# Up-projections by one level of Strassen's scheme over blocks of 384 tokens, with token-major down-projections weighted by a scalar

## The chip, the cores and the metric

The program runs on one core of a Trainium2 chip, as one launch from the inputs in the chip's memory (HBM) to the output there. A core has TensorE (PE; its weight loads are listed apart, PEld), VectorE (DVE), ScalarE (ACT), GpSimd (POOL) and SyncE (SP, which here only issues DMAs). Each engine works its own queue in order and waits for the others by semaphores. The metric is the device time in microseconds, the median of several runs.

## The reference

Three steps, all in float32; the output has 1536 tokens (2 x 768) by 512 features.

```python
# 1. attention: 2 batches, 8 heads, 768 tokens, head dimension 64; window of 128 and 4 sink tokens
scores = q @ k.T / sqrt(64)
keep = (pos_k < 4) | ((rel >= 0) & (rel < 128))        # rel = pos_q - pos_k
a = softmax(where(keep, scores, -1e9))
x = (a @ v), heads side by side: 1536 x 512
# 2. four experts, 512 -> 1024 -> 512, all of them for every token
p = domain_probs / (domain_probs.sum(-1) + 1e-9)
out = sum over e of p[:, e] * (relu(x @ w1[e]) @ w2[e])
# 3. second layer, 512 -> 2048 -> 512
h = out @ w_in
result = (h * cos(h)) @ w_out
```

## The kernel before

**Precision.** TensorE takes the reduced float32 form (fp32r) in one pass. Each operand of a projection is split into a high part, a cast (`x_hi`, `w1_hi`, `h_hi`, `w2_hi`), and a low part, the exact remainder (`x_lo` and so on), and each product is three matmuls: high x high, high x low, low x high.

**Attention.** 12 tiles of 128 tokens, 4 pairs of heads each, so `NP` = 48 steps j. Per step: scores on TensorE, masking and row maximum on VectorE (L624, L640), exponential on ScalarE (L491), normalising on VectorE (L679), a transpose of the weights, a split into two triangles on GpSimd (L386, L389), and the product with the values. The result of a tile is copied to `x_full` (L480) and split into `x_hi` (ScalarE) and `x_lo` (GpSimd L376). Between these steps the same queues load and split the first expert's weights: SP issues 256 KB of w1 and 256 KB of w2 for each of 8 chunks between the loads of keys, queries and values (`load_weights`, L276 and L279), VectorE casts w1 (L740), ScalarE casts w2, GpSimd takes both low parts.

**Projections.** A unit is one expert (1024 hidden features) or half of the second layer: `UNITS` = 6. Each unit has `STEPS` = 24 steps, 3 groups of 512 tokens by 8 chunks of 128 hidden features. In step s `up` computes one bank of 128 features x 512 tokens by 12 matmuls (4 parts of the contraction x 3, L962 to L964), two steps ahead (`LAG`), in three rotating banks. ScalarE writes `h_hi` with relu (L512), VectorE `h_lo` (L748), and `down_expert` adds 12 matmuls (L1013 to L1015: feature-major result, weights stationary) to four banks. After 8 chunks, VectorE multiplies each bank by the routing weight of each token, spread over all partitions in `probs_wide` (L775, into `routed`), and GpSimd adds it to `acc` (L433). `probs_wide` comes by a store of the routing to memory and a broadcast load of 3 MB.

**Second layer.** The same with `down` (L1032 to L1035, token-major: `h` is stationary) and a gate in place of relu: h/(2 pi) + 0.25 on ScalarE (L594, `turns`), rounding and its subtraction on VectorE (L804, L807, `frac`), sine on ScalarE (L602, `cosine`), product with h on VectorE (L819, `gated`), high part on ScalarE (L598), low part on VectorE (L812). `acc` of the experts is feature-major already and is only split into `x_hi` (L581) and `x_lo` (L440). The results are added to `acc` (L784) and stored, 12 x 256 KB (L331).

**Weights.** The next unit's chunks are loaded into four raw buffers each and split in the last third of a unit: high parts on ScalarE (L567, L571), w1's low parts on GpSimd (L424), w2's on VectorE (L761).

**Order.** Every queue is written out by hand. TensorE's is, per step, `up(u, s + LAG)` and then the down part of step s. Nothing is scheduled at run time.

## Time and profile before

| | us |
|---|---|
| runs | 917.54, 918.05, 912.59; median 917.54 |
| the profiled execution, first to last instruction | 918.1 |
| attention, until the matmuls of the projections run densely | 0 to 137 |
| expert projections | 137 to about 650 |
| second layer | about 650 to 915 |
| last accumulation and store | 915 to 918.1 |

All times are microseconds unless marked ns. Matmuls are pipelined and their records overlap, so what counts is the distance between their starts. The clock rows give the granted TensorE clock, full being 2.4 GHz and 0.5 being 1.2 GHz. Where two rows of the profile name an engine after "<-", that one ended the wait.

### The profile page before, as it was taken

To read this page: it belongs to the slowest core of one execution; us is meant where nothing else is said; L and a number is where in the kernel's file an instruction comes from. 1 tells how busy PE (TensorE), PEld (TensorE's weight loads), DVE (VectorE), ACT (ScalarE), POOL (GpSimd) and SP (SyncE) were. 2 spreads that over 40 slices of the span, in tenths; PEclk is the share of its full clock that TensorE was granted. 3 is DMA by queue.
4 is the path that set the end of the run, shared out by engine and by line. 5 is a ranking of instruction groups with operands and counts; after the bars stand their busy time and mean duration, and the time that the engine had idled before them with its cause. 6 is when DMAs were issued, how large, how long until landed. Compare 5 with 4: busy or idle time off the path is not lost.

```text
span 918.1 us, 12079 instructions
## 1 busy us (share of the span) xinstructions
PE 896.5 (98%) x4414; PEld 728.4 (79%) x4414; DVE 391.8 (43%) x892; ACT 277.0 (30%) x634; POOL 205.0 (22%) x226
## 2 busy tenths in 40 slices
PE   7889899999999999999999999999999999999998
PEld 5666578888888888888888888888788888888886
DVE  5887941312341213331214322133555456645454
ACT  5766641111221112311112211213343345333332
POOL 2564732103220204220204121235320012000000
PEclk9887989999999999999999999999999999999999
DMA  8355306000230000320001310002300002001011
GB/s 179 77 134 131 84 13 230 1 1 12 72 101 0 0 0 21 104 57 0 0 11 46 91 35 1 0 12 69 92 12 0 1 12 81 1 0 46 1 47 46
DMA packets 75020, 41.81 MB, mean 46 GB/s; under 512 B 42464, under 2 KB 67040, under 8 KB 74848
## 3 DMA queue, kind: packets, MB, share of 16 engines
q1 hardware_dynamic: 74976, 41.23, 16.4%
q8 instruction: 26, 0.43, 0.2%
q14 instruction: 18, 0.15, 0.1%
HBM read 37.79 MB, written 3.17 MB: 45 GB/s over the span
## 4 chain that ended last, share of the span: by engine, by line
PE 92%; DVE 5%; issue 1%; DMA 1%; ACT 0%; SPq 0%; ACTq 0%
PE scores L962 14%; PE scores L964 14%; PE scores L963 14%; PE bank L1015 9%; PE bank L1014 9%; PE bank L1013 9%; PE bank L1032 5%; PE bank L1035 5%; PE bank L1034 5%; DVE weights L679 2%; PE scores L899 2%; PE bank L933 2%; DVE scores L624 1%; PE bank L910 1%; DMA k_nat<-in_k_dram 1%
## 5 line engine op out<-in xcount | busy, mean ns | idle before, releaser
L962 PE MATMUL scores<-x_hi,w_hi 128*128 128x512 f32 x576 | 224.6, 390 | 0.0
L964 PE MATMUL scores<-x_hi,w_lo 128*128 128x512 f32 x576 | 224.1, 389 | 0.0
L963 PE MATMUL scores<-x_lo,w_hi 128*128 128x512 f32 x576 | 224.1, 389 | 0.0
L748 DVE SCALAR_TENSOR_TENSOR h_lo<-scores,h_hi 128x512 fp32r<-128x512 f32 x96 | 66.3, 691 | 361.4 <-ACT h_hi L512 361.4
L512 ACT ACTIVATE h_hi<-scores 128x512 fp32r<-128x512 f32 x96 | 57.4, 598 | 415.6 <-PE scores L964 415.6
L1013 PE MATMUL bank<-h_hi,w_hi 128*128 128x512 f32 x384 | 149.4, 389 | 0.0
L1014 PE MATMUL bank<-h_lo,w_hi 128*128 128x512 f32 x384 | 149.4, 389 | 0.0
L1015 PE MATMUL bank<-h_hi,w_lo 128*128 128x512 f32 x384 | 149.4, 389 | 0.0
L962 PEld LDWEIGHTS scores<-x_hi,w_hi 128*128 128x128 f32 x576 | 108.1, 188 | 22.7 <-issue 0.5
L964 PEld LDWEIGHTS scores<-x_hi,w_lo 128*128 128x128 f32 x576 | 108.2, 188 | 22.5
L963 PEld LDWEIGHTS scores<-x_lo,w_hi 128*128 128x128 f32 x576 | 108.1, 188 | 22.4
L424 POOL TENSOR_TENSOR w_lo<-w_raw,w_hi 128x512 fp32r<-128x512 f32 x40 | 51.5, 1289 | 276.9 <-ACT w_hi L567 276.9
L433 POOL TENSOR_TENSOR acc<-acc,routed 128x512 f32<-128x512 f32 x48 | 62.3, 1329 | 194.1 <-DVE routed L775 194.1
L1013 PEld LDWEIGHTS bank<-h_hi,w_hi 128*128 128x128 f32 x384 | 72.1, 188 | 15.0
L1014 PEld LDWEIGHTS bank<-h_lo,w_hi 128*128 128x128 f32 x384 | 72.1, 188 | 15.0
L1015 PEld LDWEIGHTS bank<-h_hi,w_lo 128*128 128x128 f32 x384 | 72.0, 188 | 14.9
L1032 PE MATMUL bank<-w_hi,h_hi 128*128 128x512 f32 x192 | 75.0, 391 | 0.0
L1035 PE MATMUL bank<-w_hi,h_lo 128*128 128x512 f32 x192 | 74.7, 389 | 0.0
L1034 PE MATMUL bank<-w_lo,h_hi 128*128 128x512 f32 x192 | 74.7, 389 | 0.0
L804 DVE TENSOR_SCALAR frac<-turns 128x512 f32<-128x512 f32 x48 | 21.3, 444 | 110.2 <-ACT turns L594 110.2
L594 ACT ACTIVATE turns<-scores 128x512 f32<-128x512 f32 x48 | 28.7, 598 | 129.5 <-PE scores L964 129.5
L491 ACT ACTIVATE weights<-masked,neg_max 128x132 f32<-128x132 f32 (+1 forms) x96 | 38.0, 397 | 38.7 <-DVE neg_max L640 37.5
(93 smaller groups left out, 931.5 us busy)
## 6 DMA issues: line engine op xcount, KB each, us to landing
w_raw<-in_moe_w_dram SPq DMA_DIRECT2D x64, 256.0 KB, 2.9
w_raw<-in_moe_w_in_dram SPq DMA_DIRECT2D x16, 256.0 KB, 3.1
w_raw<-in_moe_w_out_dram SPq DMA_DIRECT2D x16, 256.0 KB, 2.7
v_nat<-in_v_dram SPq DMA_DIRECT2D x12, 256.0 KB, 3.1
probs_wide<-routing_dram SPq DMA_DIRECT2D x1, 3072.0 KB, 11.3
out_dram<-acc SPq DMA_DIRECT2D x12, 256.0 KB, 2.1
k_nat<-in_k_dram SPq DMA_DIRECT2D x11, 256.0 KB, 5.0
q_nat<-in_q_dram SPq DMA_DIRECT2D x11, 256.0 KB, 5.4
```

The costliest lines, as they stand in the source:

```text
L433: nc.gpsimd.tensor_tensor(acc[:, g, c], acc[:, g, c], routed[:, c], ALU.add)\
L512: nc.scalar.activation(h_hi[:, s % U_BANKS, :], up_bank[s % U_BANKS][:], ACT.Relu)\
L748: nc.vector.scalar_tensor_tensor(h_lo[:, s % U_BANKS, :], up_bank[s % U_BANKS][:], 0.0, h_hi[:, s % U_BANKS, :].bitcast(F32), ALU.max, ALU ...
L962: nc.tensor.matmul(ub[:], w1_hi[:, f, c, :], x_hi[:, c, rows], start=(c == 0), stop=False)
L963: nc.tensor.matmul(ub[:], w1_hi[:, f, c, :], x_lo[:, c, rows], start=False, stop=False)
L964: last = nc.tensor.matmul(ub[:], w1_lo[:, f, c, :], x_hi[:, c, rows], start=False, stop=(c == KC - 1))
L1013: nc.tensor.matmul(down_bank[c][:], w2_hi[:, f, feats], h_hi[:, slot], start=(f == 0), stop=False)
L1014: nc.tensor.matmul(down_bank[c][:], w2_hi[:, f, feats], h_lo[:, slot], start=False, stop=False)
L1015: last = nc.tensor.matmul(down_bank[c][:], w2_lo[:, f, feats], h_hi[:, slot], start=False, stop=(f == FC - 1))
L1032: nc.tensor.matmul(down_bank[i][:], h_hi[:, slot, toks], w2_hi[:, f], start=(f == 0), stop=False)
L1034: nc.tensor.matmul(down_bank[i][:], h_hi[:, slot, toks], w2_lo[:, f], start=False, stop=False)
L1035: last = nc.tensor.matmul(down_bank[i][:], h_lo[:, slot, toks], w2_hi[:, f], start=False, stop=(f == FC - 1))
```

## The change

**Tiling.** The work is cut into `NS` = 24 stages of 768 tokens (one batch) and 512 hidden features: block 0 is the experts over batch 0 (stages 0 to 7), block 1 the experts over batch 1 (8 to 15), blocks 2 and 3 the second layer over batch 0 (16 to 19) and batch 1 (20 to 23), called gated stages.

**Up-projection.** In a stage, x (512 x 768) and w1 (512 x 512) are 2 x 2 matrices of blocks, 384 tokens being half the token side. Seven block products in Winograd's form of Strassen's scheme replace eight. A stage has two halves, a and b (h = 2s, 2s + 1), each of 128 of the 256 features of a block; `product(h, n)` is one of the seven for a half: 6 matmuls of 384 columns. The sums of weight blocks are made on GpSimd (`sum_weights`, 4 of 512 elements per partition and stage), those of token blocks too (`sum_tokens`, 4 of 768 per block of stages). The sums of products are made by letting products accumulate in a bank one after another (`chain_bank`: 1, 6, 5, 3; `side_bank`: 7, 4; `two_bank`: 2), and by copying the bank in between to SBUF on ScalarE (`keep_1`, `keep_2`, `keep_3` into `kept`) and adding the copy on VectorE to another bank or into `c22` (`add_11`, `add_22`, `add_21`). The next product into the chain bank waits for the copy. Each half yields four quarters, 11, 22, 12, 21, of 128 features x 384 tokens, which go through relu or the gate in pieces of 384 columns. `kept` and `c22` exist once: `keep_2(h)` waits until `add_21(h - 1)` is done.

**Down-projection.** Always token-major, as 6 tiles of 128 tokens x 512 features; `down(s, k, i)` is 6 matmuls for tile `DOWN_ORDER[k]` from half i, 72 matmuls per stage. It waits for the low parts of two quarters of its half. VectorE then adds each tile to `acc` (`keep_down`), for experts times the routing weight as a scalar per partition. The routing broadcast, its store and GpSimd's additions are gone.

**Between the layers.** `acc` is token-major now, so TensorE transposes it for the second layer (`turn_down`, 12 tiles x 4, at the ends of stages 8 to 10 and 16 to 18), VectorE copies the result to `x_t`. All seven token blocks of the next block of stages are split at the end of stages 7, 15 and 19 (`tokens_hi` on ScalarE and `tokens_lo` on VectorE, 7 x 768 columns each). The attention stage no longer splits x per tile; instead, the four token sums of batch 0 and their splits run one per step j from 30 to 42, and the weight sums and splits of stage 0 from 12 to 22 (splits of x and w1 on GpSimd and ScalarE).

**Weights.** Loads are 1 MB each, w1 and w2 once per stage, behind the stage before's last split. In an expert stage ScalarE splits the next stage's w1 after `relu_hi(b, 12)` and at the end, in a gated stage after the seventh cosine and at the end; w2 is split in the same stage (`second_hi`, `second_lo`, 2 x 1024 columns).

The diff cut to its core (helpers, names and the unchanged attention left out):

```diff
+        chain_bank = (bank[0], bank[3])
+        side_bank = (bank[1], bank[4])
+        two_bank = (bank[2], bank[5])
+        down_bank = (bank[6], bank[7], bank[2], bank[0], bank[1], bank[5])
+        x2_bank = (bank[6], bank[7])
...
-            def load_weights(first, second, u, f):
-                if not (isinstance(u, int) and RAW > u * FC + f):
-                    sp.wait_ge(w1_lo_ready, u * FC + (f - RAW + 1))
-                sp.dma_start(w1_raw[:, f % RAW], first).then_inc(w1_landed[f % RAW], 16)
-                if not (isinstance(u, int) and RAW > u * FC + f):
-                    sp.wait_ge(w2_lo_ready, u * FC + (f - RAW + 1))
-                sp.dma_start(w2_raw[:, f % RAW], second).then_inc(w2_landed[f % RAW], 16)
...
+            def load_first(s):
+                if s >= 1:
+                    sp.wait_ge(w1_lo_ready, 6 * s)
+                sp.dma_start(w1_raw[:], weights_of(s)[0].rearrange("(k p) f -> p k f", p=P)).then_inc(w1_landed, 16)
+            def load_second(s):
+                if s >= 1:
+                    sp.wait_ge(w2_lo_ready, 2 * s)
+                sp.dma_start(w2_raw[:], weights_of(s)[1].rearrange("(c p) d -> p c d", p=P)).then_inc(w2_landed, 16)
...
+            def sum_weights(s, n):
+                low, high = slice(0, FS // 2), slice(FS // 2, FS)
+                a11, a12 = w1_raw[:, 0:2, low], w1_raw[:, 2:4, low]
+                a21, a22 = w1_raw[:, 0:2, high], w1_raw[:, 2:4, high]
+                s2, s3, s4 = (w1_sum[:, i] for i in range(3))
+                if n == 0:
+                    pool.wait_ge(w1_landed, 16 * (s + 1))
+                    if s >= 1:
+                        pool.wait_ge(w1_lo_ready, 6 * s)
+                    nc.gpsimd.tensor_tensor(s3, a11, a21, ALU.subtract).then_inc(w1_summed, 1)
+                elif n == 1:
+                    pool.wait_ge(w1_summed, 4 * s + 1)
+                    nc.gpsimd.tensor_tensor(a21, a21, a22, ALU.add).then_inc(w1_summed, 1)
+                elif n == 2:
+                    pool.wait_ge(w1_summed, 4 * s + 2)
+                    nc.gpsimd.tensor_tensor(s2, a21, a11, ALU.subtract).then_inc(w1_summed, 1)
+                else:
+                    pool.wait_ge(w1_summed, 4 * s + 3)
+                    nc.gpsimd.tensor_tensor(s4, a12, s2, ALU.subtract).then_inc(w1_summed, 1)
...
+            for s in range(NS):
+                if s + 1 < NS:
+                    for n in range(4):
+                        sum_weights(s + 1, n)
+                if s + 2 in FIRST[1:3] or s + 1 == FIRST[3]:
+                    for n in range(4):
+                        sum_tokens(block_of(s) + 1, n)
+                if s + 1 < NS:
+                    for h in (2 * s + 2, 2 * s + 3):
+                        for part in range(3):
+                            first_lo(h, part)
...
+            def keep_2(h):
+                act.wait_ge(product_done[6], h + 1)
+                if h >= 1:
+                    act.wait_ge(c21_ready, h)
+                nc.scalar.activation(kept[:, 1], chain_bank[h % 2][:, 0:HALF], ACT.Copy).then_inc(kept2, 1)
...
+            def gated_hi(n):
+                h, c = 2 * FIRST[2] + n // 4, (11, 22, 12, 21)[n % 4]
+                act.wait_ge(gated_ready, n + 1)
+                act.wait_ge(down_done, TPB * (h // 2))
+                nc.scalar.activation(h_part(h_hi, h % 2, c), gated[:, n % 2], ACT.Copy).then_inc(hi_ready[c], 1)
...
+                a, b = 2 * s, 2 * s + 1
+                n = 8 * (s - FIRST[2])
+                if s >= 1:
+                    keep_1(a)
+                second_hi(s, 0)
+                if s >= 1:
+                    keep_2(a)
+                if is_gated(s):
+                    turn(n)
+                    keep_3(a)
+                    cosine(n)
+                    keep_1(b)
+                    turn(n + 1)
+                    gated_hi(n)
+                    cosine(n + 1)
+                    second_hi(s, 1)
+                    turn(n + 2)
+                    gated_hi(n + 1)
+                    cosine(n + 2)
+                    keep_2(b)
+                    turn(n + 3)
+                    gated_hi(n + 2)
+                    cosine(n + 3)
+                    turn(n + 4)
+                    keep_3(b)
+                    gated_hi(n + 3)
+                    cosine(n + 4)
+                    for m in range(n + 5, n + 8):
+                        turn(m)
+                        gated_hi(m - 1)
+                        cosine(m)
+                        if s + 1 < NS and m == n + 6:
+                            for part in range(3):
+                                first_hi(a + 2, part)
+                    gated_hi(n + 7)
+                else:
+                    relu_hi(a, 11)
+                    keep_3(a)
+                    keep_1(b)
+                    relu_hi(a, 22)
...
+                else:
+                    relu_hi(a, 11)
+                    keep_3(a)
+                    keep_1(b)
+                    relu_hi(a, 22)
+                    second_hi(s, 1)
+                    relu_hi(a, 12)
+                    keep_2(b)
+                    relu_hi(a, 21)
+                    relu_hi(b, 11)
+                    keep_3(b)
+                    relu_hi(b, 22)
+                    relu_hi(b, 12)
+                    for part in range(3):
+                        first_hi(a + 2, part)
+                    relu_hi(b, 21)
+                if closes(s):
...
+            def add_21(h):
+                dve.wait_ge(product_done[4], h + 1)
+                dve.wait_ge(kept2, h + 1)
+                c = side_bank[h % 2][:, 0:HALF]
+                nc.vector.tensor_tensor(c, c, kept[:, 1], ALU.add).then_inc(c21_ready, 1)
...
+            def fraction(n):
+                dve.wait_ge(turns_ready, n + 1)
+                nc.vector.tensor_scalar(whole[:], turns[:, n % 2], ROUND, ROUND, ALU.add, ALU.subtract)\
+                    .then_inc(rounded, 1)
+                dve.wait_ge(rounded, n + 1)
+                nc.vector.tensor_tensor(turns[:, n % 2], turns[:, n % 2], whole[:], ALU.subtract)\
+                    .then_inc(frac_ready, 1)
...
+            def keep_down(s, k):
+                n = tokens_of(s) * TPB + DOWN_ORDER[k]
+                e = expert_of(s)
+                dve.wait_ge(down_done, TPB * s + k + 1)
+                if e is None and s in FIRST:
+                    kept_one = nc.vector.tensor_copy(acc[:, n], down_bank[k][:])
+                elif e is None:
+                    kept_one = nc.vector.tensor_tensor(acc[:, n], down_bank[k][:], acc[:, n], ALU.add)
+                elif s in FIRST:
+                    kept_one = nc.vector.tensor_scalar(acc[:, n], down_bank[k][:], probs[:, n, e:e + 1], None, ALU.mult)
+                else:
+                    kept_one = nc.vector.scalar_tensor_tensor(acc[:, n], down_bank[k][:], probs[:, n, e:e + 1],
+                                                              acc[:, n], ALU.mult, ALU.add)
+                kept_one.then_inc(down_kept, 1)
...
+                a, b = 2 * s, 2 * s + 1
+                n = 8 * (s - FIRST[2])
+                second_lo(s, 0)
+                add_11(a)
+                if is_gated(s):
+                    fraction(n)
+                    add_22(a)
+                    gate(n)
+                    fraction(n + 1)
+                    gated_lo(n)
+                    gate(n + 1)
+                    second_lo(s, 1)
+                    fraction(n + 2)
+                    gated_lo(n + 1)
+                    gate(n + 2)
+                    add_21(a)
+                    fraction(n + 3)
+                    gated_lo(n + 2)
+                    gate(n + 3)
+                    add_11(b)
+                    fraction(n + 4)
+                    gated_lo(n + 3)
+                    gate(n + 4)
+                    add_22(b)
+                    fraction(n + 5)
+                    gated_lo(n + 4)
+                    gate(n + 5)
+                    fraction(n + 6)
+                    gated_lo(n + 5)
+                    gate(n + 6)
+                    add_21(b)
+                    fraction(n + 7)
+                    gated_lo(n + 6)
+                    gate(n + 7)
+                    gated_lo(n + 7)
+                else:
+                    relu_lo(a, 11)
...
+                elif n == 6:
+                    target, first = chain_bank[i], False
+                    pe.wait_ge(kept1, h + 1)
+                elif n == 5:
+                    target, first = chain_bank[i], False
+                    pe.wait_ge(kept2, h + 1)
+                elif n == 3:
+                    target, first = chain_bank[i], False
+                    pe.wait_ge(kept3, h + 1)
+                else:
+                    target, first = side_bank[i], False
+                    pe.wait_ge(c22_ready, h + 1)
+                slot = W_SLOT[n]
...
+                slot = W_SLOT[n]
+                for d in range(2):
+                    nc.tensor.matmul(target[:, 0:HALF], w1_hi[:, i, slot, d], x_hi[:, n - 1, d],
+                                     start=first and d == 0, stop=False, skip_group_check=True)
+                    nc.tensor.matmul(target[:, 0:HALF], w1_hi[:, i, slot, d], x_lo[:, n - 1, d],
+                                     start=False, stop=False, skip_group_check=True)
+                    last = nc.tensor.matmul(target[:, 0:HALF], w1_lo[:, i, slot, d], x_hi[:, n - 1, d],
+                                            start=False, stop=d == 1, skip_group_check=True)
+                last.then_inc(product_done[n], 1)
...
+            for s in range(NS):
+                a, b = 2 * s, 2 * s + 1
+                if s >= 1:
+                    for n in PRODUCTS[:5]:
+                        product(a, n)
+                product(b, 1)
+                product(b, 7)
+                product(a, 3)
+                product(b, 6)
+                product(a, 4)
+                product(b, 2)
+                product(b, 5)
+                down(s, 0, 0)
+                product(b, 3)
+                down(s, 1, 0)
+                down(s, 2, 0)
+                product(b, 4)
+                for k in range(3, TPB):
+                    down(s, k, 0)
+                for k in range(TPB):
+                    down(s, k, 1)
+                for i in range(len(turned_tiles(s))):
+                    turn_down(s, i)
```

## Rows read from the trace of the kernel before

**Rows 1.** the page: the engines' busy time, and TensorE's clock in 40 slices.
```profile
PE 896.5 (98%) x4414; PEld 728.4 (79%) x4414; DVE 391.8 (43%) x892; ACT 277.0 (30%) x634; POOL 205.0 (22%) x226
PEclk9887989999999999999999999999999999999999
```

**Rows 2.** groups by line: engine, operation, shapes, count, busy us, mean ns, idle before.
```profile
L962 PE MATMUL scores<-x_hi,w_hi 128*128 128x512 f32 x576 | 224.6, 390 | 0.0
L1013 PE MATMUL bank<-h_hi,w_hi 128*128 128x512 f32 x384 | 149.4, 389 | 0.0
L1032 PE MATMUL bank<-w_hi,h_hi 128*128 128x512 f32 x192 | 75.0, 391 | 0.0
L964 PEld LDWEIGHTS scores<-x_hi,w_lo 128*128 128x128 f32 x576 | 108.2, 188 | 22.5
```

**Rows 3.** timeline of TensorE, dense stretch: start us, length us, engine, line, operation.
```profile
199.73 0.39 PE L1015 MATMUL bank<-h_hi,w_lo 128*128 128x512 f32 x1
...
202.90 0.39 PE L963 MATMUL scores<-x_lo,w_hi 128*128 128x512 f32 x1
```

**Rows 4.** busy time by windows: us, busy (count) by engine, clock, DMA share, GB/s.
```profile
150.00:640.00 490.00, 490.00 (x2164) 405.73 (x2163) 135.08 (x161) 87.50 (x156) 105.66 (x81) 1.00 0.11 33
```

**Rows 5.** timeline of the weight loads of the sink product, 128 columns wide.
```profile
32.34 0.52 PEld L947 LDWEIGHTS bank<-sink_t,v_sink 96*128 96x128 f32 x4 [0.17 <-issue]
```

**Rows 6.** the chain that ended last, in order of time: start us, us, what.
```profile
31.35 0.48 PE bank L853 x4
...
61.00 1.67 DVE weights L679 x2
...
66.32 7.04 DMA k_nat<-in_k_dram
```

**Rows 7.** groups by line, the other engines (columns as in rows 2).
```profile
L424 POOL TENSOR_TENSOR w_lo<-w_raw,w_hi 128x512 fp32r<-128x512 f32 x40 | 51.5, 1289 | 276.9 <-ACT w_hi L567 276.9
L775 DVE TENSOR_TENSOR routed<-bank,probs_wide 128x512 f32<-128x512 f32 x48 | 47.9, 1059 | 0.0
L594 ACT ACTIVATE turns<-scores 128x512 f32<-128x512 f32 x48 | 28.7, 598 | 129.5 <-PE scores L964 129.5
L499 ACT ACTIVATE weights_t<-bank 128x256 f32<-128x256 f32 x48 | 17.3, 361 | 1.9 <-PE bank L910 1.9
L640 DVE CUSTOM_DVE_ANT_0 masked<-scores,mask 128x132 f32<-128x132 f32 x64 | 16.4, 293 | 1.1
```

**Rows 8.** timeline of VectorE, then ScalarE, in the second layer.
```profile
760.91 0.69 DVE L807 TENSOR_TENSOR frac<-turns,frac 128x512 f32<-128x512 f32 x1
761.52 0.68 DVE L812 TENSOR_TENSOR h_lo<-gated,h_hi 128x512 fp32r<-128x512 f32 x1
...
761.64 0.63 ACT L602 ACTIVATE cosine<-frac 128x512 f32<-128x512 f32 x1 [0.70 <-DVE frac L807]
...
762.18 0.62 ACT L567 ACTIVATE w_hi<-w_raw 128x512 fp32r<-128x512 f32 x1
762.70 0.61 ACT L571 ACTIVATE w_hi<-w_raw 128x512 fp32r<-128x512 f32 x1
```

**Rows 9.** one line's instructions: duration ns min/median/max, first and last start.
```profile
L761 DVE TENSOR_TENSOR w_lo<-w_raw,w_hi x35: 679/1361/1370, 233.1 to 790.1; 128x512 fp32r<-128x512 f32 x35
...
L804 DVE TENSOR_SCALAR frac<-turns x48: 415/427/1274, 651.3 to 907.3; 128x512 f32<-128x512 f32 x48
...
L748 DVE SCALAR_TENSOR_TENSOR h_lo<-scores,h_hi x96: 690/691/693, 137.3 to 645.5; 128x512 fp32r<-128x512 f32 x96
```

**Rows 10.** busy time by windows, attention stage (columns as in rows 4).
```profile
74.80:88.50 13.70, 13.70 (x79) 9.75 (x79) 9.20 (x42) 7.70 (x26) 5.71 (x8) 0.50 0.48 110
115.80:122.60 6.80, 6.80 (x45) 4.80 (x44) 4.17 (x24) 4.03 (x16) 1.68 (x5) 0.50 0.17 40
```

**Rows 11.** timeline of TensorE before the clock fell at 115.8.
```profile
114.24 0.44 PE L910 MATMUL bank<-ident,weights 128*128 128x128 f32 x2 [1.37 <-DVE weights L679]
```

**Rows 12.** the page: DMA issues, KB each, us from issue to landing.
```profile
out_dram<-acc SPq DMA_DIRECT2D x12, 256.0 KB, 2.1
```

734 lines of the change are left out of this document (377 added, 357 removed).

## Prediction

> **What bounds the kernel now.** I read the page's engine table first: TensorE is busy 98% of the span, VectorE 43%, ScalarE 30%, GpSimd 22%; its clock row shows drops only in the first sixth [rows 1]. The list of groups by line then gives the work: 576 x 3 up matmuls, 384 x 3 expert down matmuls, 192 x 3 in the second layer, all 512 columns wide, 3456 in all [rows 2]. The timeline of TensorE shows how they follow one another: 14 starts between 199.73 and 202.90 us, 0.2264 us apart, and the same distance (490/2164) over 490 us [rows 3, 4]. The 0.39 us of a single matmul is its length, not its spacing; a result is there about 0.39 - 0.23 = 0.16 us after the next could begin. So 3456 x 0.2264 = 782.4 us of 918.1 are this stream, without a gap, and the other engines wait for it. What shortens the stream pays, until another engine has to be waited for.
>
> **The matmuls.** One stage (768 tokens x 512 hidden features) now costs 144 x 0.2264 = 32.6 us. After: 84 up matmuls of 384 columns (2 halves x 7 products x 2 x 3) and 72 down matmuls of 512. No dense stream of 384 columns is in the trace. At the full clock 512 columns are 213 ns, which leaves 13 ns fixed; 384 give 160 + 13 = 173 ns. Below it is 0.75 x 226 = 170. Above it is 188, the duration of a weight load, if loads could not overlap each other; but four loads of this size before 128-column matmuls take 0.52 us together, (0.52 - 0.19)/3 = 0.11 apart [rows 2, 5], so loads don't set it. I take 173. A stage is 84 x 0.173 + 72 x 0.2264 = 14.5 + 16.3 = 30.8 us; 24 stages 740.0, that is **-42.4**. The turned second input adds 12 groups of four transposes, 0.48 us for four by the key transposes [rows 6], a little less behind one another: **+5**.
>
> The Trainium skill ("TensorE: Matmul & The Clock Gate", Back-to-back issue gap) gives N/2.4 + 2.5 ns between matmuls. At 512 columns that is 216 and the row says 226, so the row decides; by the page 384 columns would be 162.5 ns, and 1344 of them in the stages where TensorE sets the end would bring the sum to about 939.
>
> **The other engines: durations.** ScalarE takes 361 ns for 256 and 598 for 512 columns, so 480 for 384. VectorE takes 293 for 132 and 691 for 512, so 557 for 384; its rounding 427 for 512, taken as 370. Behind one another without dependence they overlap by 0.1 (ScalarE) and 0.08 (VectorE), and a handoff between engines takes 0.04 [rows 7 to 9].
>
> **An expert stage (16 of 24).** New are six additions and copies of product sums per stage: 6 x 0.48 on ScalarE, 6 x 0.56 on VectorE, and on GpSimd 4 weight sums and 6 low parts, some 14 us by 1.29 for 512 columns [rows 7]. All sums stay below 30.8, so only dependences count. The tightest: product 4 of half a lands at 10.5 us of the stage, add_21 0.56, keep_2 of half b 0.48, handoffs 0.12: 11.7, and product 5 of half b wants it at 11.4. That is 0.3 per stage. The lead of the others is longer: relu_lo(a,12) ends near 10, wanted at 12.5. At a block's end seven 768-column splits (0.96 each, up to twice that with GpSimd at work) stand between the six accumulations, which end 1 to 2 us late. Together **+8**.
>
> **A gated stage (8 of 24).** Here I lay the four queues side by side, from the stage's start. Products 1, 7, 6, 2 end at 4.15 and land at 4.3; add_11 ends at 4.9, turn at 5.4. From there each quarter is a round trip: round 0.37, fraction 0.56, sine 0.48, gate 0.56 and four handoffs, 2.1 us, and VectorE's queue lets the rounding of the next begin only behind the gate. Between them stand add_22(a) (0.5), then second_hi and second_lo of 1024 columns (1.1 and 1.2, VectorE waits for the first), so the sines end at 6.9, 9.2, 12.9 and the third gate at 13.5. Only then comes add_21(a), 13.9, and ScalarE has **keep_2 of half b behind the third cosine and behind that sum**: 14.5. Product 6 of half b had landed at 9.5 and product 5 should start at 11.4: it starts at 14.6, and everything of half b behind it in TensorE's queue waits too. Then the quarters go on: 4 more rounds with add_11(b), add_22(b), add_21(b) and the three weight splits on ScalarE (2.0) between, and the low part of quarter 12 of half b is there at 28.2. Its six down matmul groups should start at 22.7. So the stage ends at 28.3 + 6 x 1.36 = 36.5 instead of 30.8. Nothing of it is caught up: the next stage's gating can't begin before its own products, which stand behind those down matmuls. The last stage lacks the weight splits. Stages of 37.3 (with turns) three times, 39 at the block's end, 36.5 three times, 36.0: **+47** over 8 x 30.8.
>
> **What GpSimd adds there.** A subtraction of two SBUF inputs on VectorE takes 679 ns alone and 1361 with GpSimd at work, the 427 ns rounding up to 1274; relu_lo, one input from PSUM, stays at 690 to 693 in all 96 [rows 9]. In a gated stage the weight sums of the next stage meet the first fraction (+0.8) and the three low parts (4.5 us) the last rounding and fraction (+2). That is 0 to +3.5 per stage and 5 more where the token sums run; I take most of it, **+22** (bounds 0 and 27). The Trainium skill ("GPSIMD Engine Reference", Specifications) says the SBUF interfaces are shared with VectorE for 2-port modes and two SBUF inputs; the trace agrees with 679 against 1361, and the rule speaks against a change that moves sums to GpSimd.
>
> **The attention stage and the ends.** 4 MB of weights in 8 pairs of loads no longer stand in SP's queue between key loads, with the routing store; only 1 + 1 MB do. A key load took 7.04 us at 66.32 [rows 6], and TensorE then ran 13.7 us at half clock [rows 10]. VectorE loses 8 casts of about the rounding's 0.43. Against that, GpSimd gets 21 sums and subtractions of 1.3 to 1.9 us for 27 of 1.3, eleven of them one behind each pair of heads, beside its selects; the normalising of VectorE waits for such an operation (1.67 us for two [rows 6]). Bounds -9 and +5; I take **-4**. Behind the last matmul nothing changes: 0.7 for the last accumulation, 2.1 to store [rows 12]. The removed routing multiply (1.06, x48 [rows 7]) and GpSimd's additions lay under the matmuls and give nothing; the scalar form takes their place at 0.7 from PSUM, 96 times, under the last six down groups of each stage, 1.36 apart. Without that cover it would be 0.7 a stage, the last one. The DMAs of 1 MB have a whole stage to land; the copy of routing to all partitions is gone, 11 us that nobody waited for.
>
> **Sum.** 918.1 (the profiled execution; the median of the runs is 917.5) - 42.4 + 5 + 8 + 47 + 22 - 4 = 953.6: **953 us**.
>
> **Rivals.** (1) *The gating is hidden*: TensorE never waits and the matmul saving arrives: 918.1 - 42.4 + 5 + 8 - 4 = 885. For it: VectorE has 8 x 2.05 + 6 x 0.56 + 2 x 1.2 + 6 x 0.7 = 26 us and ScalarE some 21 us of work in 30.8. Against it: the round trips are in sequence, and 28.2 lies far behind 22.7. It decides when a round takes 0.2 us less and GpSimd costs nothing: then the wait falls from 5.9 to 4.2 per stage and the change is even; below 908 it needs as much again. Chance 0.07. (2) *Round trips as reckoned or slightly quicker, GpSimd out of the way* (its sums fall where VectorE reads PSUM): 915 to 927, chance 0.13. (3) *The clock falls in the new gaps.* TensorE would stand 3 to 4 us before product 5 and 1 to 3 before half b's downs. In the attention stage its clock went to 0.50 for 6.8 us at 115.8 after an idle of 1.37 [rows 10, 11]. Behind the first gap the slower matmuls are hidden by the round trips; behind the second, 6.8 us at half speed cost 3.4: 8 x 3.4 = 27, giving 980. Against it: around the gaps the stream is dense. Chance 0.12. The Trainium skill ("TensorE: Matmul & The Clock Gate", Why this matters for your kernels) warns of such gaps between bursts of matmuls. (4) *384 columns don't come at 173 but at 188*: in the 16 expert stages 84 x 0.015 = 1.3 each, 21 in all, mostly hidden in gated ones: 973, within the range.
>
> **Numbers.** Forecast (928 to 975) 0.68, clock 0.12, even 0.13, hidden 0.07. Range: from just below the forecast's lower end (GpSimd at 0: 931, pitch 170 and attention -9: 922) to the clock case, 925 to 980. A difference of 1% is about what can be measured here: faster 0.07, within 1% 0.13, slower 0.80.
>
> **What would show it.** Up matmuls 0.173 apart; expert stages of 31 us, gated ones of 37 to 41; TensorE's waits led by keep_2 (copy of product 6, ScalarE) and by the low parts of the gated values; the two-input fraction with a maximum near 1.1 us; TensorE's busy share below 95% in the last third. I am wrong if product 5 of half b starts without a wait in gated stages, if ScalarE or VectorE operations of 384 columns are much shorter than 480 and 557 ns, or if the half clock shows up in the last third.

## The result, and the profile after

| | us | ratio to before (95%) |
|---|---|---|
| before | 917.59 (912.59 to 918.05) | |
| after | 1003.94 (1000.02 to 1006.19) | 1.0951 (1.0908 to 1.0995) |
| forecast | 953 (925 to 980) | |

The change costs 9.5%. The forecast had the sign right, but it said 3.9%, and the time lies outside its range. These are lines of the page of the changed kernel, to be read beside [rows 1]: the engines' busy us, share of the span and number of instructions; then TensorE's clock in 40 slices; then the chain of work that ended last, by engine.

```profile
span 1002.5 us, 14172 instructions
PE 902.6 (90%) x4750; PEld 781.2 (78%) x4750; DVE 608.8 (61%) x1235; ACT 445.1 (44%) x966; POOL 434.5 (43%) x360
PEclk9979799999999998999999999989999988889899
...
PE 71%; DVE 16%; issue 6%; ACT 6%; DMA 0%; ACTq 0%; DVEq 0%
```

TensorE is no longer busy throughout: 90% for 98%. No other engine is full either. What it waits for is a chain of dependent work on the others (the chain row has 22% on VectorE and ScalarE). GpSimd is busy for 434.5 us instead of 205.0, more than twice as long.

Three stretches of the same profile follow: six expert stages (1 to 6), the last eight stages (gated), and stage 19 alone, the last of block 2 (columns as in [rows 4]).

```profile
166.00:356.50 190.50, 188.23 (x938) 168.61 (x937) 90.31 (x132) 72.57 (x132) 96.97 (x65) 1.00 0.21 67
...
657.80:1000.00 342.20, 280.87 (x1272) 245.33 (x1272) 244.41 (x383) 157.34 (x306) 113.34 (x74) 0.92 0.15 50
786.20:835.10 48.90, 34.09 (x160) 29.57 (x158) 41.20 (x55) 24.53 (x45) 24.14 (x14) 0.92 0.07 22
```

In the six expert stages TensorE works 188.2 of 190.5 us. In the gated stages it idles for 61 of 342 us. From the first matmul of a stage to the first of the next, stages last (us):

| stages | forecast | measured |
|---|---|---|
| start of stage 1 | 159.3 | 166.0 |
| 1 to 5 | 31 | 31.65 each |
| 6, 7, 8, 9 | 31 to 33 | 32.2, 35.4, 35.1, 32.5 |
| 10 to 13 | 31 | 32.5, 31.7, 31.65, 31.65 |
| 14, 15 | 31 to 33 | 35.4, 35.4 |
| 16 to 23, gated | 36 to 41 | 43.6, 41.05, 43.75, 48.8, 45.7, 41.0, 41.0, 36.5 |

(159.3: the old stream of 782.4 us ended at 914.9, so it stands as if begun at 132.5; -4 for the attention stage, + 30.8 for stage 0.)

### The profile page after: what moved, and what is told of

Its sections match the earlier page's. It is cut to its first block, busy times and chain, and to the rows that moved or that the text cites. A ratio compares the mean times of both kernels' runs of the same rounds, so it can differ in the third digit from the quotient of the medians.

```text
span 1002.5 us, 14172 instructions
## 1 busy us (share of the span) xinstructions
PE 902.6 (90%) x4750; PEld 781.2 (78%) x4750; DVE 608.8 (61%) x1235; ACT 445.1 (44%) x966; POOL 434.5 (43%) x360
## 3 DMA queue, kind: packets, MB, share of 16 engines
HBM read 59.81 MB, written 3.15 MB: 63 GB/s over the span
## 4 chain that ended last, share of the span: by engine, by line
PE 71%; DVE 16%; issue 6%; ACT 6%; DMA 0%; ACTq 0%; DVEq 0%
PE scores L1159 9%; PE scores L1163 8%; PE scores L1161 8%; PE bank L1192 7%; PE bank L1194 7%; PE bank L1196 6%; PE scores L1192 6%; PE scores L1194 6%; PE scores L1196 6%; DVE turns L911 2%; DVE x_lo L873 2%; DVE weights L804 2%; DVE whole L908 2%; DVE scores L898 1%; PE bank L1161 1%
## 5 line engine op out<-in xcount | busy, mean ns | idle before, releaser
L451 POOL TENSOR_TENSOR w_lo<-w_raw,w_hi 128x512 fp32r<-128x512 f32 x96 | 128.2, 1336 | 342.2 <-ACT w_hi L570 341.6
L1159 PE MATMUL scores<-x_hi,w_hi 128*128 128x384 f32 x528 | 187.1, 354 | 59.1 <-ACT kept L600 41.6
L1161 PE MATMUL scores<-x_lo,w_hi 128*128 128x384 f32 x528 | 183.0, 347 | 0.0
L1163 PE MATMUL scores<-x_hi,w_lo 128*128 128x384 f32 x528 | 182.7, 346 | 0.0
L1192 PE MATMUL scores<-w_hi,h_hi 128*128 128x512 f32 x288 | 113.2, 393 | 0.0
L1194 PE MATMUL scores<-w_lo,h_hi 128*128 128x512 f32 x288 | 113.0, 392 | 0.0
L1196 PE MATMUL scores<-w_hi,h_lo 128*128 128x512 f32 x288 | 112.3, 390 | 0.0
L867 DVE TENSOR_TENSOR w_lo<-w_raw,w_hi 128x1024 fp32r<-128x1024 f32 x48 | 69.0, 1438 | 55.3 <-ACT w_hi L578 55.3
L451 POOL TENSOR_TENSOR w_lo<-w_sum,w_hi 128x768 fp32r<-128x768 f32 x48 | 90.8, 1892 | 0.0
L1194 PEld LDWEIGHTS bank<-w_lo,h_hi 128*128 128x128 f32 x288 | 57.2, 199 | 9.7
L639 ACT ACTIVATE gated<-turns 128x384 f32<-128x384 f32 x64 | 33.6, 525 | 68.2 <-DVE turns L911 68.2
```

Of the source, the lines that this page charges most:

```text
L451: nc.gpsimd.tensor_tensor(w1_slots(w1_lo, h % 2, part), w1_part(h % 2, part), w1_slots(w1_hi, h % 2, part).bitcast(F32), ALU.subtract)\
L639: nc.scalar.activation(gated[:, n % 2], turns[:, n % 2], ACT.Sin, scale=TWO_PI)\
L867: nc.vector.tensor_tensor(w2_lo[:, i::2], w2_raw[:, i::2], w2_hi[:, i::2].bitcast(F32), ALU.subtract)\
L1159: nc.tensor.matmul(target[:, 0:HALF], w1_hi[:, i, slot, d], x_hi[:, n - 1, d], start=first and d == 0, stop=False, skip_group_check=True)
L1161: nc.tensor.matmul(target[:, 0:HALF], w1_hi[:, i, slot, d], x_lo[:, n - 1, d], start=False, stop=False, skip_group_check=True)
L1163: last = nc.tensor.matmul(target[:, 0:HALF], w1_lo[:, i, slot, d], x_hi[:, n - 1, d], start=False, stop=d == 1, skip_group_check=True)
```

## The matmuls and one gated stage, row by row

TensorE's timeline in an expert stage, which answers to [rows 3]: start us, length us.

```profile
199.75 0.33 PE L1159 MATMUL scores<-x_hi,w_hi 128*128 128x384 f32 x1
199.93 0.33 PE L1161 MATMUL scores<-x_lo,w_hi 128*128 128x384 f32 x1
...
203.22 0.33 PE L1163 MATMUL scores<-x_hi,w_lo 128*128 128x384 f32 x1
203.39 0.33 PE L1159 MATMUL scores<-x_hi,w_hi 128*128 128x384 f32 x1
```

The 21 distances from 199.75 to 203.39 take 3.64 us: 0.173 us each, the term of the forecast to the nanosecond. By the Trainium skill ("TensorE: Matmul & The Clock Gate", Back-to-back issue gap), the estimate would have been 384/2.4 + 2.5 = 162.5 ns; the row decides, as it did at 512 columns. The 512-column matmuls of the new down-projections came 0.226, 0.229 and 0.232 apart in turn, 0.229 in the mean, 2.6 ns more than before.

Now one gated stage, 17, which starts at 701.5: TensorE, then ScalarE, then TensorE again (the bracket is the idle time before, and what ended it).

```profile
713.05 0.34 PE L1163 MATMUL bank<-x_hi,w_lo 128*128 128x384 f32 x1
717.26 0.41 PE L1159 MATMUL scores<-x_hi,w_hi 128*128 128x384 f32 x1 [3.87 <-ACT kept L600]
...
714.95 0.52 ACT L639 ACTIVATE gated<-turns 128x384 f32<-128x384 f32 x1 [1.37 <-DVE turns L911]
716.63 0.49 ACT L600 ACTIVATE kept<-scores 128x384 f32<-128x384 f32 x1 [1.16 <-DVE scores L898]
...
730.50 0.40 PE L1196 MATMUL bank<-w_hi,h_lo 128*128 128x512 f32 x1
733.37 0.47 PE L1192 MATMUL bank<-w_hi,h_hi 128*128 128x512 f32 x1 [2.47 <-issue]
```

This is the place the forecast named: product 5 of half b waits for `keep_2` (L600), which stands behind the third cosine (L639) and behind `add_21` (L898). It starts at 15.8 of the stage (forecast 14.6 without GpSimd), and the down groups of half b begin at 31.9 (28.3 without). What made both later is VectorE beside GpSimd in the same stage:

```profile
704.25 1.56 DVE L867 TENSOR_TENSOR w_lo<-w_raw,w_hi 128x1024 fp32r<-128x1024 f32 x1 [1.50 <-ACT w_hi L578]
707.42 1.52 DVE L911 TENSOR_TENSOR turns<-turns,whole 128x384 f32<-128x384 f32 x1
729.53 1.74 DVE L908 TENSOR_SCALAR whole<-turns 128x384 f32<-128x384 f32 x1 [1.12 <-ACT turns L630]
731.30 1.50 DVE L911 TENSOR_TENSOR turns<-turns,whole 128x384 f32<-128x384 f32 x1
...
704.81 2.15 POOL L440 TENSOR_TENSOR w_raw<-w_raw 128x512 f32<-128x512 f32 x1
707.04 1.49 POOL L443 TENSOR_TENSOR w_sum<-w_raw 128x512 f32<-128x512 f32 x1
729.20 1.85 POOL L451 TENSOR_TENSOR w_lo<-w_sum,w_hi 128x768 fp32r<-128x768 f32 x1
731.01 1.38 POOL L451 TENSOR_TENSOR w_lo<-w_raw,w_hi 128x512 fp32r<-128x512 f32 x1
```

Read it by who started first. L867 had begun at 704.25 when GpSimd's L440 started at 704.81: GpSimd's took 2.15 for 1.29, and ended 1.15 after VectorE's. L443 started at 707.04, and the fraction L911 behind it took 1.52 where it takes 0.56 alone: it ended at 708.94, 0.41 after GpSimd's. L451 began at 729.20 and ended at 731.05; the rounding L908, 0.36 alone, began at 729.53 and ended at 731.27. The one that comes second stands until the other has ended; only 0.14 or 0.15 us of its own duration (0.36 less 0.22, 0.56 less 0.41) lie before that.

These are the minimum, median and maximum of the fraction and the rounding over all 64 quarters, in ns, first in the changed kernel:

```profile
L911 DVE TENSOR_TENSOR turns<-turns,whole x64: 557/559/2086, 666.5 to 989.7; 128x384 f32<-128x384 f32 x64
L908 DVE TENSOR_SCALAR whole<-turns x64: 345/360/1752, 666.1 to 989.3; 128x384 f32<-128x384 f32 x64
```

and then in e2 below, where GpSimd's operations are cut to a few columns:

```profile
L916 DVE TENSOR_TENSOR turns<-turns,whole x64: 557/558/561, 654.2 to 939.7; 128x384 f32<-128x384 f32 x64
L913 DVE TENSOR_SCALAR whole<-turns x64: 351/360/364, 653.8 to 939.3; 128x384 f32<-128x384 f32 x64
```

At the end of a block there is more of it. Stage 14, where GpSimd makes the token sums of the next block:

```profile
594.43 2.24 DVE L902 SCALAR_TENSOR_TENSOR h_lo<-c,h_hi 128x384 fp32r<-128x384 f32 x1 [0.84 <-ACT h_hi L624]
596.60 2.86 DVE L867 TENSOR_TENSOR w_lo<-w_raw,w_hi 128x1024 fp32r<-128x1024 f32 x1
...
594.41 1.85 POOL L472 TENSOR_TENSOR x_t<-x_t 128x768 f32<-128x768 f32 x1
596.34 2.04 POOL L475 TENSOR_TENSOR t_sum<-x_t 128x768 f32<-128x768 f32 x1
598.45 2.67 POOL L478 TENSOR_TENSOR t_sum<-x_t,t_sum 128x768 f32<-128x768 f32 x1
```

Both lose in turn: 0.56 becomes 2.24 and 1.23 becomes 2.86, then GpSimd's 1.83 becomes 2.67. Over the whole run, `relu_lo` is hit only in the quarter 22, whose two inputs both lie in SBUF (`c22`); from PSUM it never is:

```profile
L902 DVE SCALAR_TENSOR_TENSOR h_lo<-scores,h_hi x64: 544/557/559, 140.8 to 638.6; 128x384 fp32r<-128x384 f32 x64
L902 DVE SCALAR_TENSOR_TENSOR h_lo<-c,h_hi x32: 558/559/2240, 142.4 to 637.4; 128x384 fp32r<-128x384 f32 x32
```

## Experiments

Medians are of several runs each. The kernel before took 919.65 on the chip of e1 to e4, 917.51 on that of e5 to e8 and 916.61 on that of e9 to e11. Ratios are to those, and differences between kernels are worked out from the ratios times 917.6.

**e1: without the gate.** All stages use the path of the experts; the gate is left out.

```diff
     def is_gated(s):
-        return s >= FIRST[2]
+        return False
```

> The changed kernel with the gate of the second layer left out: stages 16 to 23 apply relu, in the queue orders of the expert stages (the output is not the reference's). Theory A (the gated stages are set by the round trips between ScalarE and VectorE): stages 16 to 23 fall from 341.5 us to about the 266 us that stages 8 to 15 take in the trace after, so about 1002 - 75 = 927 us. Rival B (the loss lies in what all Strassen stages share: weight sums, copies, half clock): the gated stages lose less than 30 us, 970 or more.

Measured: 930.58, ratio 1.012 (1.0084 to 1.0156). The last eight stages lasted 35.2, 32.55, 32.5, 36.4, 34.4, 31.6, 31.65 and 31.8, together 266.1 for 341.5. The round trips of the gate, with what is held up in them, cost 76 us, and the rival that looked for the loss elsewhere (970 or more) falls.

**e2: GpSimd almost idle.** From stage 1 on its sums and low parts are cut to 4 or 8 columns; the rest of them is left out.

```diff
+                if s >= 1:
+                    a11, a12, a21, a22, s2, s3, s4 = (v[:, :, 0:8] for v in (a11, a12, a21, a22, s2, s3, s4))
...
+                cols = slice(0, P if h < 2 else 4)
...
+                if b >= 1:
+                    b11, b12, b21, b22, t2, t3, t4 = (v[:, :, 0:8] for v in (b11, b12, b21, b22, t2, t3, t4))
```

> The changed kernel, but from stage 1 on GpSimd's sums and low parts cover 4 or 8 columns of each block instead of 128 to 384: every wait and order stands, the work is left out (the output is not the reference's). Theory A (a two-input SBUF operation of VectorE all but stands still while GpSimd's runs, 2.24 us for 0.56): expert stages stay near 31.6, the stages at a block's end fall from 35.4 to about 32, gated ones from 41 to about 37.5; with fewer falls of the clock 945 us. Rival (VectorE is only slowed to half, as I had reckoned): -25 to -30, 973 us. Rival (contention is nothing): 1002.

Measured: 953.87, ratio 1.0373 (1.033 to 1.0417), 53 us less than after and 9 more than theory A expected. Its stages: 31.65 up to 13 and in 14 (but 32.2 to 32.5 in 7 to 10 and 15), gated 38.5, 37.8, 37.8, 39.3, 37.1, 36.9, 37.3, 36.5. In its second gated stage (from 686.7):

```profile
701.56 0.44 PE L1164 MATMUL scores<-x_hi,w_hi 128*128 128x384 f32 x1 [3.15 <-ACT kept L605]
715.35 0.47 PE L1197 MATMUL bank<-w_hi,h_hi 128*128 128x512 f32 x1 [0.50 <-issue]
```

Product 5 of half b starts at 14.9 and half b's downs at 28.6: the forecast's 14.6 and 28.3, worked out for exactly this case. So the gated chain had been sized rightly, and what GpSimd adds had not. The experiment takes more away than GpSimd's hold on VectorE. GpSimd's own time goes too, but that isn't what TensorE waited for: stages 1 to 5 last 31.65 in both kernels, and at the head of a block TensorE waits for VectorE (below). And TensorE's clock is at its lower level for 31 us after stage 0 here, for 68 in the changed kernel.

**e3: the copy of product 6 kept per half**, and taken before the third cosine.

```diff
-        kept = sb("kept", [P, 3, HALF])
+        kept = sb("kept", [P, 4, HALF])
...
-                if h >= 1:
-                    act.wait_ge(c21_ready, h)
-                nc.scalar.activation(kept[:, 1], chain_bank[h % 2][:, 0:HALF], ACT.Copy).then_inc(kept2, 1)
+                if h >= 2:
+                    act.wait_ge(c21_ready, h - 1)
+                nc.scalar.activation(kept[:, (1, 3)[h % 2]], chain_bank[h % 2][:, 0:HALF], ACT.Copy).then_inc(kept2, 1)
...
                     second_hi(s, 1)
+                    keep_2(b)
                     turn(n + 2)
                     gated_hi(n + 1)
                     cosine(n + 2)
-                    keep_2(b)
```

> The changed kernel with a buffer of its own for the copy of product 6 in each half, so that keep_2 of half b doesn't wait for add_21 of half a, and with keep_2(b) two quarters earlier in ScalarE's queue. The 4 us wait before product 5 of half b goes. Theory A (the chain of quarters sets the stage, the wait before half b's downs grows by what the first loses): expert stages 0.4 us less each, gated ones under 1, together -8 to -14, 990 us. Rival (the place of that copy is the cause): -4 x 8 - 6 = -38, 964 us.

Measured: 984.04, ratio 1.0716 (1.0678 to 1.0755): 22 us less, between theory A's 8 to 14 and the rival's 38. Of that, 12.5 us lie in stages 1 to 15 and 8 in the gated ones. An expert stage fell from 31.65 to 31.11, the 0.54 us by which product 5 of half b had waited there. In a gated stage (from 687.2) TensorE's waits are now these:

```profile
704.34 0.77 PE L1192 MATMUL bank<-w_hi,h_hi 128*128 128x512 f32 x1 [4.01 <-DVE h_lo L923]
718.65 0.47 PE L1192 MATMUL bank<-w_hi,h_hi 128*128 128x512 f32 x1 [2.18 <-issue]
```

The wait before product 5 is gone and a wait of 4.0 stands before the first down group instead, for the low part of half a. The stage is 40.6 for 41.05. What sets it is the sequence of eight round trips, and `keep_2` is only where that first shows.

**e4: TensorE kept busy in the gaps** by idle matmuls into free banks: 20 before product 5 of half b in gated stages, 18 where a block opens.

```diff
+            def fill(target, count, still, moving):
+                for _ in range(count):
+                    nc.tensor.matmul(target[:, 0:HALF], still, moving,
+                                     start=True, stop=True, skip_group_check=True)
```

> The changed kernel with idle matmuls in TensorE's gaps: 18 of 384 columns before the first product of stages 8, 16 and 20, and 20 before product 5 of half b in each gated stage, into banks that are free (their sums are never read). The half clock, 57 us of the stages after 127 in the trace, should mostly go. Theory A (in gated stages the slow matmuls are hidden by the round trips, only those behind a block's end cost): -8 to -14, 991 us. Rival (half of the time at half clock is lost wherever it falls): -28, 974 us. Rival (costs nothing): 1002.

Measured: 999.81, ratio 1.0884 (1.0846 to 1.0921). The mean granted clock rose from 0.952 to 0.977 and the time fell by 6 us (4 by the medians), less than the 8 to 14 of theory A. Where the half clock was not hidden it shows: stage 8, from its first product on, went from 35.1 to 32.5. But the filling took away only part of the half clock, 68 us after stage 0 (the 57 of the expectation are those of the gated stages) becoming 28, and part of what was left fell where it isn't hidden: half b's downs took 9.7 to 10.9 us for 8.1 in stages 16, 20, 21 and 22, in the changed kernel only in 18 and 20. So 6 us is a net gain and not the price of all the half clock. An estimate of that price, from stages of the changed kernel that ran at either clock: 2.6 us at the head of each of stages 8, 16 and 20 and 1.6 in half b's downs of 18 and 20, some 11 in all; the rest hides behind the round trips.

**e5 and e9: only the down-projections changed.** The kernel before, with token-major expert downs and the routing weight as a scalar. In e5 VectorE waits at the top for GpSimd's clearing of `acc`; e9 moves that wait to the first addition.

```diff
-                return nc.vector.tensor_tensor(routed[:, c], down_bank[c][:],
-                                               probs_wide[:, g * 512:(g + 1) * 512, u], ALU.mult)
+                return nc.vector.scalar_tensor_tensor(acc[:, g, i], down_bank[i][:], probs[:, g * GT + i:g * GT + i + 1, u],
+                                                      acc[:, g, i], ALU.mult, ALU.add)
```

> The kernel before with only the second part of the change: experts' down-projections token-major, the routing weight as a scalar on VectorE straight into acc, without the routing broadcast, its store and GpSimd's additions. The turn of acc for the second layer is left out (its output is not the reference's; in the changed kernel it costs 12 x 0.4 = 5 us). Theory A (this part lies under the matmuls and costs nothing): 915 to 919 us. Rival (adding in one VectorE operation holds up the banks or the next group): over 925.

Measured: 923.78, ratio 1.0072 (1.0046 to 1.0097), outside the 915 to 919 expected. Its dense stretch ran at 0.2267 a matmul, like before; the loss is one wait that the experiment itself put there, 6.7 us of it on TensorE:

```profile
140.67 0.06 DVE L778 MEMSET probs_sum<- 128x1 f32 x1 [11.60 <-POOL acc L409]
```

> The kernel before with its expert down-projections made token-major (the turn and the transposes are left out, so the values are not the reference's), as in the run of that kind before, with one wait moved: VectorE no longer awaits GpSimd's clearing of the accumulator (5.2 us) at the top of the projections but at the first addition. Theory A: that wait was all of the 6 us by which the earlier form was slower; its dense stretch ran at 0.2267 a matmul. Then 917 us, 1.000 of before. Theory B: the scalar form or the token-major order costs something of its own: above 921.

Measured: 913.70, ratio 0.9968 (0.9935 to 1.0001), 3 us under the 917 expected. Without the wait this part of the change is even, or a few us better.

**e6: plain products in the gated stages**, Strassen's scheme for the experts only, with e3's copy. The core of the edit; without product sums, each gated quarter is one accumulation, and the copies and additions leave the round trips' queues.

```diff
+            def quarter(h, c):
...
+                pairs = ((1, 2), (5, 3))[c % 10 - 1]
+                for k, n in enumerate(pairs):
+                    slot = 2 * (c // 10 - 1) + k
+                    for d in range(2):
+                        nc.tensor.matmul(target[:, 0:HALF], w1_hi[:, i, slot, d], x_hi[:, n - 1, d],
+                                         start=k == 0 and d == 0, stop=False, skip_group_check=True)
...
-                if s + 1 < NS:
+                if s + 1 < FIRST[2]:
                     for n in range(4):
                         sum_weights(s + 1, n)
```

> The changed kernel with Strassen's scheme for the experts only and eight plain block products in the second layer's stages: no copies, no additions and no weight or token sums there, quarters ready from 2.3 us of the stage on instead of 4.9, and the separate copy of product 6 of e3 in the expert stages. TensorE has 96 x 0.173 + 72 x 0.2264 = 32.9 us per gated stage instead of 30.8. Theory A (the gate fits when it starts earlier and has no additions between): no waits in gated stages, 8 x 33.3, start of stage 16 at 642: 915 us, just below the kernel before. Rival (the round trips and GpSimd still set them): 38 and more per gated stage, above 950.

Measured: 915.12, ratio 0.9971 (0.9951 to 0.9991), as expected. The gated stages last 33.2 to 34.3 for 36.5 to 48.8, though each has 12 more matmuls. Part of that is GpSimd: without the sums none of its operations meets the gate's, and the fraction is never held up here, where it had reached 2086 ns:

```profile
L920 DVE TENSOR_TENSOR turns<-turns,whole x64: 557/559/561, 645.2 to 899.9; 128x384 f32<-128x384 f32 x64
```

Against e2's gated stages (36.5 to 39.3), which are free of it too, the plain ones are 3 to 5 us shorter.

**e7: the splits of the next tokens earlier** in stages 7 and 15, before `relu_hi(b, 21)` and `add_21(b)`.

```diff
                     relu_lo(b, 12)
+                    if closes(s):
+                        for i in range(early(s, 5)):
+                            tokens_lo(block_of(s) + 1, i)
                     add_21(b)
```

> e6 with the splits of the next block's tokens in stages 7 and 15 moved ahead: six high parts on ScalarE before the weight splits, five low parts on VectorE before add_21 of half b, where VectorE waits for product 4 anyway. Theory: the wait of 3.7 us before stage 8 goes and with it the half clock behind it (2 us): 5 us less than e6, 910. Rival (they collide with GpSimd's low parts there instead and delay relu's last quarter): no gain.

Measured: 910.41, ratio 0.9927 (0.9897 to 0.9958). Stage 7 fell from 34.9 to 31.7 and stage 8 from 33.5 to 32.0. This is the best kernel of the study, 7 us below the kernel before, with the interval clear of 1.

**e8: in the attention stage, the first tokens' sums and splits at every second step** instead of every step, on e7.

```diff
-                if 30 <= j < 34:
-                    sum_tokens(0, j - 30)
-                if 36 <= j < 43:
-                    split_first_tokens(j - 36)
+                if 29 <= j < 36 and j % 2:
+                    sum_tokens(0, (j - 29) // 2)
+                if 37 <= j < 50 and j % 2:
+                    split_first_tokens((j - 37) // 2)
```

> e7 with GpSimd's four sums and seven splits of the first tokens in the attention stage one for every second pair of heads (steps 29 to 49) instead of one for each (30 to 42). In the trace after, attention's steps run 5 us ahead of before at step 32 and 4 behind at step 44. Theory A (crowded GpSimd operations hold up the normalising on VectorE): 3 to 6 us less than e7. Rival (each such operation costs the same wherever it is): the same as e7.

Measured: 913.42, ratio 0.9964 (0.9939 to 0.9988). There is no gain, rather a loss of 3 (the two intervals overlap). Stage 1 starts at 167.0 for 166.1. Spreading the operations changes neither their number nor what each can hold up.

**e10: the same operations cut to 8 columns** (so that the first tokens' sums and low parts are left out), on the changed kernel.

```diff
+                if b == 0:
+                    b11, b12, b21, b22, t2, t3, t4 = (v[:, :, 0:8] for v in (b11, b12, b21, b22, t2, t3, t4))
...
-                nc.gpsimd.tensor_tensor(x_lo[:, n - 1], x_block(0, n), x_hi[:, n - 1].bitcast(F32), ALU.subtract)\
+                nc.gpsimd.tensor_tensor(x_lo[:, n - 1][:, :, 0:8], x_block(0, n)[:, :, 0:8],
+                                        x_hi[:, n - 1].bitcast(F32)[:, :, 0:8], ALU.subtract)\
```

> The changed kernel with GpSimd's eleven operations for the first tokens in the attention stage (four sums, seven low parts) cut to 8 of 384 columns, so the first stages' low parts and sums are left out; the rest of the two fields is cleared beforehand, one piece per step between steps 20 and 29. Theory A: these eleven hold VectorE's two-input operations up, and that is why the attention stage is 7 us later than forecast and falls behind from its ninth tile on: stage 1 then starts near 159 instead of 166 and the time is 997. Theory B: it is the transfers and the clock, not GpSimd: stage 1 at 164 to 166, 1002 to 1004.

Measured: 997.08, ratio 1.0864 (1.0797 to 1.093). The time is theory A's, but the profile bears out only a part of it: stage 1 starts at 162.7, not at 159. Nor is the experiment clean: its ten clearings of GpSimd (0.74 us each) hold the normalising up as well, by up to 2.553 us for 0.28, and the ninth tile's scores begin at 89.4 for 81.6. Five profiled executions with the attention stage of after untouched (after, e1, e2, e4, e11) start stage 1 at 163.5 to 169.6, 167.4 in the mean, so one execution settles this to a few us only. The attention stage's excess stays open.

**e11: e1 and e2 together**, no gate and GpSimd almost idle.

> The changed kernel without the gate (relu in the last eight stages) and with GpSimd's operations cut to 4 or 8 columns from stage 1 on: both left-out parts of the two earlier runs in one. Theory A: both only removed waits, so all stages but those at a block's ends run at 31.65 and stage 1 starts at 166 to 169: 169 + 23 x 31.65 + 3 x 1.5 for the block ends = 901, plus 3 behind the last matmul = 904. Theory B: there is a further wait in the last stages, for instance the turned tiles or the 1 MB loads: above 912.

Measured: 906.92, ratio 0.9899 (0.9869 to 0.9929); 904 was expected, and the rival's 912 is not reached. Stages last 31.65 except 32.1 to 32.5 at block ends and where tiles are turned. From e2 to e11 the gate alone, with GpSimd out of the way, costs (1.0373 - 0.9899) x 917.6 = 43 us: 47 had been forecast. From e1 to e11, GpSimd costs 20 us where there is no gate.

## Why the prediction was right, and where it was not

Its terms against the stages of the profiled executions. "Without GpSimd" is e2.

| term | forecast | measured |
|---|---|---|
| start of stage 1 | 159.3 | 166.0: +6.7 |
| stages 1 to 15 without GpSimd | 15 x 30.8 + 8 + 2.5 (turns) = 472.5 | 478.6: +6.1 |
| gated stages without GpSimd | 296.4 | 301.1: +4.7 |
| GpSimd | 22 | 13.2 + 40.4 = 53.6: +31.6 |
| sum | 953.6 | 953.6 + 49.1 = 1002.7; the execution took 1002.5 |

**Right: the matmuls.** 173 ns at 384 columns, and the stream did shorten. The rival of 188 ns is out. A stage without waits is 31.1 (e3) and not 30.8, mostly because the downs came at 229 and not 226.4 ns (72 x 2.6 = 0.2 us).

**Right: an expert stage sets no great wait.** `keep_2` of half b behind `add_21` was named as the tightest, at 0.3; e3 shows 0.54. With the 229 ns it makes most of the +6.1.

**Right: the gated stage.** The place, the cause and the size came out: 14.9 and 28.6 us of the stage where 14.6 and 28.3 had been worked out, 43 us by e2 and e11 where 47 were forecast. It was a sum over queues laid side by side, and it held to a third of a microsecond. The rival in which the gate is hidden (885) needed round trips shorter than any row allowed.

**Wrong: "what GpSimd adds", bounds 0 and 27, taken at 22.** This term failed, and 53.6 was measured. Three things were missing in it: how much one operation loses, what happens at the ends of blocks, and the clock. The first is a reading of [rows 9]: 679 ns alone and 1361 "with GpSimd at work" was taken as an operation running at half speed, so that it could lose little more than its own length (the fraction was to show "a maximum near 1.1 us"; it was 2.09). The pair behind that row, VectorE and GpSimd of the kernel before, reads otherwise:

```profile
646.55 1.36 DVE L761 TENSOR_TENSOR w_lo<-w_raw,w_hi 128x512 fp32r<-128x512 f32 x1 [0.35 <-ACT w_hi L571]
...
646.07 1.29 POOL L424 TENSOR_TENSOR w_lo<-w_raw,w_hi 128x512 fp32r<-128x512 f32 x1 [2.45 <-ACT w_hi L567]
```

GpSimd's ends at 647.36, and VectorE's 0.55 later: it stood still for 0.81 us and then ran. The loss is what was left of the other's operation, not a share of its own, and in this row the rest happened to be the same 0.8 nearly each time (median 1361, maximum 1370), which looked like a doubling. The rounding in the same rows, 427 ns alone and 1274 at most, was the sign: half speed can't give a factor of three. The Trainium skill states it ("SBUF — State Buffer", Who interferes with whom): the ports shared by VectorE and GpSimd are an exclusive lock, whoever issues first has them for the whole instruction, and two SBUF inputs, or a fast two-port form such as `tensor_scalar` can take, are what wants them. The traces agree: 0.36 became 1.74, and in the attention stage of the changed kernel the normalising, with one SBUF input, reached 1.868 for 0.284:

```profile
L804 DVE TENSOR_SCALAR weights<-weights,row_inv x96: 273/284/1868, 8.1 to 128.8; 128x132 f32<-128x132 f32 x80, 128x128 f32<-128x128 f32 x16
```

Counted over the trace, VectorE's operations lost 35 us to GpSimd in stages 16 to 22. With each loss held to the operation's own length it would have been 16. In the ordinary gated stages 17, 18, 21, 22 and 23, GpSimd cost 3.3, 6.0, 4.1, 3.7 and 0 us, where 0 to 3.5 had been set and some 2 taken.

The second is where the losses are paid. Around the ends of blocks 5 us had been set and 36 came: 3.2, 2.6, 3.8 and 3.2 in stages 7, 8, 14 and 15, 5.1 in 16, and 9.6 and 8.6 in 19 and 20. There GpSimd's token sums of 1.83 (stages 14 and 19) and low parts meet VectorE's short operations and its seven splits of 0.95, each of which can wait for up to 1.85; at the end of stage 7 two of them took 3.90 together:

```profile
385.61 3.90 DVE L873 TENSOR_TENSOR x_lo<-x_t,x_hi 128x768 fp32r<-128x768 f32 x2
...
384.17 2.57 POOL L451 TENSOR_TENSOR w_lo<-w_sum,w_hi 128x768 fp32r<-128x768 f32 x1
386.70 1.99 POOL L451 TENSOR_TENSOR w_lo<-w_raw,w_hi 128x512 fp32r<-128x512 f32 x1
```

Here half speed would have given the same 2 us; what was missed is that the delay is paid in full. The first product of the next block waits for the splits and for a bank whose accumulation stands between them in VectorE's queue:

```profile
391.85 0.66 PE L1159 MATMUL scores<-x_hi,w_hi 128*128 128x384 f32 x1 [3.58 <-DVE acc L938]
```

In stage 19 it is paid because the gate's chain stands behind: product 5 of half b waited 6.48 us, for 3.15 in e2's.

The third is the clock. Behind these waits TensorE's clock was at 0.50, and the fourth product of stages 8, 16 and 20 began at 5.8 to 5.9 us of the stage for 3.15. Stage 8's 2.6 is nothing else: in e4, with GpSimd's work as it was, it is gone. By the estimate at e4 some 11 of the 53.6 are half clock, which e2 doesn't have in these places.

**Wrong in size: the attention stage at -4.** It came out near +3 (166.0 for 159.3). The gain of the loads was there early: the scores of the ninth tile start at 81.6 for 86.8 before, but those of the twelfth at 119.7 for 115.8. [rows 6] had two normalisings in 1.67 us, and that was a hold-up of the same kind: they ended 0.1 behind GpSimd's split of x (61.30 to 62.57). But it doesn't explain the excess. GpSimd's operations became fewer and longer, and over all 96 the normalising took the same before and after (the last two numbers are busy us and mean ns before the idle time):

```profile
L679 DVE TENSOR_SCALAR weights<-weights,row_inv 128x132 f32<-128x132 f32 (+1 forms) x96 | 41.3, 471 | 0.0
L804 DVE TENSOR_SCALAR weights<-weights,row_inv 128x132 f32<-128x132 f32 (+1 forms) x96 | 41.9, 477 | 0.0
```

e10 gives back some 4 to 8 us, e8 nothing, and the cause of the excess stays open.

**The clock** was a rival at 980, given 0.12, on the premise that half b's downs would run at half clock in every gated stage. They did so in two of eight, 18 and 20, at 1.6 us each and not 3.4. The half clock did come, 68 us of it after stage 0 and 57 of these in the gated stages, which the prediction had named as a sign that it would be wrong. Most of it fell behind the wait before product 5, where the prediction had said that it would be hidden. What it had not looked at is the head of a block.

**Right: the parts costed at nothing.** The routing's scalar form and the token-major order gave nothing that can be told from even (e9).

## What to carry to other kernels

Where a trace shows an operation "slower beside another engine", put the two instructions side by side by their starts and ends before making a factor of it: a lock costs the rest of the holder's instruction, whatever the length of the one that waits, so short operations on a chain must be priced with the longest operation of the other engine. Moving sums to an engine that looks idle is not free if its instructions hold up the engine that carries the chain, and what they hold up at a point where TensorE then stands is paid twice, by the wait and by the clock behind it. And fewer matmuls pay only where the extra sums stay off a sequence of dependent round trips: here one level of Strassen's scheme gains in the relu stages (e7, 910.4 for 917.5) and loses 3 to 14 us per stage against plain products in the gated ones (36.5 to 48.8 for 33.2 to 34.3), 3 to 5 of it without GpSimd's share (e2).
